# A linear recurrence, a routed expert layer and a second network in one kernel: choice of experts taken into the recurrence

## The chip, the cores and the metric

One core of a Trainium2 chip runs the whole program. The metric is the device time of one execution in microseconds. Engines are written PE (TensorE), DVE (VectorE), ACT (ScalarE), POOL (GpSimd) and SP (SyncE, which here only issues DMAs).

## The reference

Three stages follow each other, with 4 batches x 768 steps = 3072 tokens of 8 heads x 48 = 384 features.

```python
def _attn_ref(q, k, v, alpha):            # q, k, v, alpha: (4, 8, 768, 48)
    for t in range(S):
        state = alpha[:, :, t, :, None] * state + einsum('bhd,bhe->bhde', k[:, :, t], v[:, :, t])
        y[:, :, t] = einsum('bhd,bhde->bhe', q[:, :, t], state)

def _moe_ref(x, expert_emb, tau, w1, w2):  # x (3072, 384), 8 experts, w1 (8, 384, 1024), w2 (8, 1024, 384)
    logits = normalised(x) @ normalised(expert_emb).T / tau
    expert_idx = argmax(logits, axis=1)
    gate_w = softmax(logits)[expert_idx]
    out[mask_e] = gate_w * (relu(x[mask_e] @ w1[e]) @ w2[e])

def _moe2_ref(x, w_in, w_out):             # w_in (384, 2048), w_out (2048, 384)
    h = x @ w_in
    return max(0.01 * h, h) @ w_out
```

## The kernel before

**Recurrence.** Tokens are cut into 24 tiles of 128 steps (6 chunks of time x 4 batches, tile n = 4 chunk + batch). Each engine runs its own program; semaphores tie them together. For a tile DVE makes the running products of alpha forward and backward (`prepare`, L788 to L796: scan, reciprocal, scan), POOL multiplies them into q and k (L517 `qt`, L522 `kt`), PE makes the scores (L1133) and turns the keys (L1139), DVE masks the scores (L804), PE multiplies with the values (L1168), makes the outer products for the state (L1188) and adds the part from the old state (L1176), DVE adds up the state (L823), POOL scales it (L530), ACT copies, PE turns the result back and projects it on the expert embeddings (L1148), ACT copies rows and logits (L625, L626) and SP stores the rows to HBM. All engines are one or two tiles apart in a fixed order: PE's step is scores of n+1, projection of n-1, values, outer products and from-state of n; DVE's is prepare of n+2, mask of n+1, state of n; POOL's is prepare of n+2, then the scaling of the state of n-1. DVE's scan of tile n+2 waits for the scaled state of n-2 (L787). The first and the last chunks are written out, those between run in a loop.

**Choice of experts.** It stands between the recurrence and the first expert matmul. When all 24 tiles are through, DVE finds for every token the largest logit (L885 to L906), PE counts and ranks the tokens of each expert (L1220, L1221), DVE lays out 31 windows of 128 slots, each window with tokens of one expert (L919 to L985), then it marks for each tile which slot a token takes (L995 to L1000), POOL multiplies gate values into the marks (L549), and PE sums the marks over the tiles, 24 matmuls (L1226), which gives for every slot its token and its gate. POOL gathers the rows of a window from HBM by these indices (L564).

**Windows.** A window's rows are turned (L1240), multiplied with w1 in two halves of 9 matmuls each (`hidden`, L1249), ReLU, turned (L1260), and multiplied with w2 in 24 matmuls (`contract`, L1269). Every operand is split into a rounded part (ACT) and a rest (DVE: L1037 for x, L1053 for h, L349 for the weights, in six pieces per expert), with three matmuls per product. DVE multiplies the result with the gate (L1065), and POOL scatters the rows to HBM (L585). PE's order is: hidden half of the next window, turn of this one's h, other hidden half, turn of the rows of the one after, contraction.

**Second network.** Rows come back from HBM, six groups of 512 tokens, L1319 and L1326.

## Time and profile before

| | us |
|---|---|
| median of three runs | 882.3 (879.5 to 883.55) |
| profiled execution | 880.55 |
| its span, first to last instruction | 878.7 |
| PE busy | 836.8 |
| PE weight loads | 751.6 |
| DVE busy | 419.7 |
| ACT busy | 334.2 |
| POOL busy | 160.1 |
| from one window's contraction to the next | 9.55 |
| DMA engines, busy share of 30 to 120 us | 0.79 to 0.91 |

Busy time of PE contains the filler matmuls of L1124, and matmul ends are modelled. "Idle before" in a row stands in brackets: how long the engine was idle and who ended it. L numbers are lines of the kernel. The timeline gives start and duration; the chain of waits follows the work that ended last back to its releasers.

### The profile page before, as it was taken

What the parts mean: (1) busy time and instruction counts of PE and PEld (TensorE: products, weight loads), DVE (VectorE), ACT (ScalarE), POOL (GpSimd) and SP (SyncE); (2) the same over time, 40 slices, a digit from 0 to 9 for tenths busy, and PEclk for the clock granted to TensorE, in tenths of its full rate; (3) what the DMA queues carried; (4) which work ended last, traced back from release to release, by engine and by line L of the source; (5) the groups of instructions that cost most, each with busy time, mean ns of one, the idle gap of its engine ahead of it and who ended that gap; (6) DMA issues with size and microseconds to landing.
All of it is one profiled execution on the core that took longest, in us unless ns stands there. A gap on an engine that the chain in (4) does not pass through costs nothing.

```text
span 878.7 us, 17061 instructions
## 1 busy us (share of the span) xinstructions
PE 836.8 (95%) x5435; PEld 751.6 (86%) x5436; DVE 419.7 (48%) x643; ACT 334.2 (38%) x624; POOL 160.1 (18%) x216
## 2 busy tenths in 40 slices
PE   7999974899999999999997999999999999999998
PEld 6888854699999999999985999998998999999997
DVE  7788849444455253455244343343343343343332
ACT  2455443334435344444333333333333333333323
POOL 5566623222222222322210000000000000000000
PEclk7999995899999999999998999999999999999999
DMA  9898860552453351553305000200200300100100
GB/s 220 200 215 207 198 207 0 180 180 65 159 179 123 103 179 32 192 179 105 106 2 107 1 1 25 49 1 6 66 0 0 72 0 0 37 1 1 37 1 36
DMA packets 45265, 76.24 MB, mean 87 GB/s; under 512 B 16231, under 2 KB 35731, under 8 KB 45232
## 3 DMA queue, kind: packets, MB, share of 16 engines
q1 hardware_dynamic: 41264, 64.98, 26.6%
q0 software_dynamic: 3968, 10.82, 3.5%
q8 instruction: 20, 0.33, 0.2%
q14 instruction: 13, 0.11, 0.0%
HBM read 61.63 MB, written 15.53 MB: 88 GB/s over the span
## 4 chain that ended last, share of the span: by engine, by line
PE 84%; issue 4%; DVE 4%; POOL 3%; DMA 2%; SPq 1%; ACT 0%; POOLq 0%; DVEq 0%
PE bank L1326 23%; PE bank L1319 23%; PE bank L1269 15%; PE bank L1249 14%; PE bank L1260 3%; POOL kt L522 1%; PE bank L1240 1%; DVE decay L788 1%; PE bank L1148 1%; PE bank L1133 1%; PE bank L1168 1%; DMA xg<-x_rows,isrc 1%; DVE inv L796 1%; POOL state L530 1%; DMA taus<-tau 1%
## 5 line engine op out<-in xcount | busy, mean ns | idle before, releaser
L1319 PE MATMUL bank<-yT,wts 128*128 128x512 f32 x864 | 217.0, 396 | 6.1 <-DVE yT L1082 6.1
L1326 PE MATMUL bank<-wts,gs 128*128 128x384 f32 x1152 | 217.3, 337 | 0.0
L1326 PEld LDWEIGHTS bank<-wts,gs 128*128 128x128 f32 x1152 | 204.4, 188 | 8.9 <-issue 0.4
L1319 PEld LDWEIGHTS bank<-yT,wts 128*128 128x128 f32 x864 | 161.9, 189 | 36.6 <-DVE yT L1082 6.9
L1100 DVE TENSOR_TENSOR g<-bank,small 128x512 f32<-128x512 f32 x96 | 66.4, 691 | 180.6 <-ACT small L743 180.6
L1249 PE MATMUL bank<-wts,gxT 128*128 (+1 forms) x558 | 143.2, 401 | 1.2 <-DVE gxT L1037 1.2
L1269 PE MATMUL bank<-wts,hT 128*128 x744 | 137.3, 339 | 1.6 <-DVE hT L1053 1.6
L1269 PEld LDWEIGHTS bank<-wts,hT 128*128 128x128 f32 x744 | 128.5, 188 | 1.9 <-issue 1.8
L743 ACT ACTIVATE small<-bank 128x512 f32<-128x512 f32 x96 | 57.3, 597 | 191.0 <-PE bank L1319 190.9
L1249 PEld LDWEIGHTS bank<-wts,gxT 128*128 128x128 f32 x558 | 103.0, 190 | 20.9 <-DVE gxT L1037 1.5
L1102 DVE TENSOR_TENSOR gs<-g,gs 128x512 fp32r<-128x512 f32 x96 | 66.4, 692 | 67.0 <-ACT gs L746 67.0
L746 ACT ACTIVATE gs<-g 128x512 fp32r<-128x512 f32 x96 | 60.7, 632 | 72.7 <-DVE g L1100 72.7
L690 ACT ACTIVATE hT<-bank 128x512 fp32r<-128x512 f32 x62 | 33.6, 595 | 126.7 <-PE bank L1260 126.7
L349 DVE TENSOR_TENSOR wts<-raw,wts 128x1024 f32 (+1 forms) x60 | 69.9, 1220 | 18.7 <-ACT wts L343 18.7
L585 POOL DMA_INDIRECT y_rows<-ys,idst x31 | 32.2, 1040 | 198.6 <-DVE ys L1065 198.6
L1053 DVE TENSOR_TENSOR hT<-bank,hT 128x512 fp32r<-128x512 f32 x62 | 39.9, 686 | 53.9 <-ACT hT L690 53.9
L343 ACT ACTIVATE wts<-raw 128x1024 f32 (+1 forms) x60 | 58.9, 1056 | 2.5 <-PE bank L1269 2.5
L1065 DVE TENSOR_SCALAR ys<-bank,slot_gate 128x384 f32<-128x384 f32 x31 | 19.0, 614 | 47.4 <-PE bank L1269 47.4
L1037 DVE TENSOR_TENSOR gxT<-bank,gxT 128x384 fp32r<-128x384 f32 x31 | 17.3, 557 | 47.6 <-ACT gxT L669 47.6
L673 ACT ACTIVATE hs<-bank 128x512 f32<-128x512 f32 x62 | 37.2, 601 | 7.1 <-PE bank L1249 7.1
L564 POOL DMA_INDIRECT xg<-x_rows,isrc x31 | 33.5, 1081 | 28.1 <-POOL isrc L558 27.0
L517 POOL TENSOR_TENSOR qt<-qkas,decay 112x512 f32<-112x512 f32 x24 | 30.6, 1275 | 40.4 <-DVE decay L788 40.4
(155 smaller groups left out, 676.9 us busy)
## 6 DMA issues: line engine op xcount, KB each, us to landing
raw<-w SPq DMA_DIRECT2D x14, 1536.0 KB, 7.1
qkas<-qka SPq DMA_DIRECT2D x40, 289.5 KB, 4.8
vs<-v SPq DMA_DIRECT2D x24, 192.0 KB, 4.7
x_rows<-xs SPq DMA_DIRECT2D x24, 192.0 KB, 4.5
yl<-y_rows SPq DMA_DIRECT2D x24, 192.0 KB, 4.4
out<-os SPq DMA_DIRECT2D x5, 768.0 KB, 4.3
raw<-w_in SPq DMA_DIRECT2D x2, 1536.0 KB, 6.8
raw<-w_out SPq DMA_DIRECT2D x2, 1536.0 KB, 7.3
```

The costliest lines, as they stand in the source:

```text
L343: act.activation(set_of(par, 0, cols), raw[:, cols], ACT.Copy).then_inc(w_hi, 1)
L349: dve.tensor_tensor(set_of(par, 1, cols), raw[:, cols], set_of(par, 0, cols).bitcast(F32), ALU.subtract).then_inc(w_lo, 1)
L673: act.activation(hs[:, u, half * HALF:(half + 1) * HALF], hps[u][half][:, :], ACT.Relu).then_inc(relu_done, 1)
L743: act.activation(small[:, f % 2], gps[f % 2][:, :], ACT.Copy, scale=0.01).then_inc(small_done, 1)
L746: act.activation(gs[:, f % 4, 0], g[:, f % 2], ACT.Copy).then_inc(g_hi, 1)
L1053: dve.tensor_tensor(hT[:, 1, h], htps[half][:, :], hT[:, 0, h].bitcast(F32), ALU.subtract).then_inc(ht_lo, 1)
L1100: dve.tensor_tensor(g[:, f % 2], gps[f % 2][:, :], small[:, f % 2], ALU.max).then_inc(g_done, 1)
L1102: dve.tensor_tensor(gs[:, f % 4, 1], g[:, f % 2], gs[:, f % 4, 0].bitcast(F32), ALU.subtract).then_inc(g_lo, 1)
L1249: m = pe.matmul(hps[u][half][:, :], gxT[:, u, x_part, k * P:(k + 1) * P], set_of(par, w_part, slice(n, n + HALF)), start=(k == 0 and (x_pa ...
L1269: m = pe.matmul(yeps, hT[:, h_part, k * P:(k + 1) * P], set_of(par, w_part, slice(n, n + D)), start=(k == 0 and (h_part, w_part) == (0, 0) ...
L1319: m = pe.matmul(gps[f % 2][:, :], wts[:, 0, w_part, n:n + P], yT[:, u, y_part, k], start=(k == 0 and (w_part, y_part) == (0, 0)), stop=(k ...
L1326: m = pe.matmul(ops[tt], gs[:, f % 4, g_part, tt * P:(tt + 1) * P], wts[:, 1, w_part, f * D:(f + 1) * D], start=(f == 0 and (g_part, w_par ...
```

## The change

The choice of experts is spread over the recurrence, and the gate moves to the end.

- The loops over tiles are written out. POOL scales the state of tile n-1 before it prepares tile n+2.
- tau goes into the embeddings, so that logits come out ready. DVE runs `route` for groups of four tiles (the last four tiles are two groups of two) at tiles 5, 9, 13, 17, 21 and after the end: best expert of each token, and a scan that counts on from the groups before. PE sums the ranks (`rank_group`), and DVE's `rank` turns them into a place in the expert's own list (3072 places per expert).
- POOL's `mark` makes two one-hot arrays per tile, 128 x 192 for the list's column and 128 x 128 for the row times token number. PE sums them over four tiles (`list_chunk`), DVE adds this to what it has (`add_listed`). The result holds each expert's tokens in columns of 128.
- After 16 tiles DVE picks the expert with most tokens (`choose_first`). Its weights are loaded first, experts follow in cyclic order, and two windows of it are sure. Their rows are gathered when the lists of 16 tiles are there, near the end of the recurrence. Turn, hidden layer and contraction of windows 0 and 1 are written out by hand between the last tiles, routes, ranks and lists.
- The layout of windows (`lay_out`, `encode`) runs on one partition. The gate is computed after the second window (`weigh`) and applied at the very end by ACT as it copies the output (scale of `os_`); DVE's L1065 becomes a plain copy.
- Tokens are stored in the order of tiles, and `o_grp` undoes it. Many tiles of the recurrence lie in the memory of the second weight set. PSUM banks 6 and 7 change roles.

```diff
-        MADE = 9
-        SLOT_TILES = 6
+        MADE = 3
+        TABLES = 13
-        START_BUSY, GATHER_BUSY, Y_BUSY = 12, 10, 26
+        START_BUSY, Y_BUSY = 12, 26
+        ROUTE_AT = {BATCHES * (g + 1) + 1: g for g in range(CH - 1)}
+        RANK_AT = {n + 1: g for n, g in ROUTE_AT.items()}
+        MARK_AT = {t + 7: (t,) for t in range(12)} | {19: (12, 13), 20: (14, 15)}
+        LIST_AT = {BATCHES * c + 11: c for c in range(3)} | {21: 3}
...
@@ sync
+            for n in range(TILES - BATCHES):
+                refill_qka(n + 2)
+                sp.wait_ge(tile_done, n + 1)
+                load_v(n + BATCHES)
+                if n > 0:
+                    store_x(n - 1)
+                if n == TILES - BATCHES - 2:
+                    sp.wait_ge(first_known, 1)
+                    expert0 = sp.value_load(est[0:1, 0:1], min_val=0, max_val=E - 1)
+                    load_first(0, expert0)
+                    load_first(1, expert0)
+            for part in range(2, PIECES):
+                load_first(part, expert0)
...
@@ gpsimd
+            def mark(t):
+                pool.wait_ge(pos_ready, group_of(t) + 1)
+                wait_from(pool, list_summed, (t - HOTS) // BATCHES + 1)
+                pool.tensor_scalar(list_hot[:, t % HOTS], list_at[:, :], pos[:, 1, t:t + 1], None,
+                                   ALU.is_equal).then_inc(list_marked, 1)
+                pool.tensor_scalar(row_hot[:, t % HOTS], row_at[:, :], pos[:, 2, t:t + 1], token[:, t:t + 1],
+                                   ALU.is_equal, ALU.mult).then_inc(list_marked, 1)
+            for n in range(TILES):
+                if 0 < n <= TILES - BATCHES:
+                    scale_state(n - 1)
+                if n + 2 < TILES:
+                    prepare(n + 2)
+                for t in MARK_AT.get(n, ()):
+                    mark(t)
+            wait_stored(SURE * BATCHES)
+            pool.wait_ge(members_ready, 1)
+            for w in range(2):
+                fetch(w, EARLY)
+            for t in range(SURE * BATCHES, TILES):
+                mark(t)
...
@@ vector
+            def route(g):
+                dve.wait_ge(lg_copied, tiles[-1] + 1)
+                dve.tensor_reduce(lg, lgq[:, r0:r0 + G], AX.X, ALU.add).then_inc(lg_summed, 1)
+                dve.tensor_copy(heads[G][:, :, 0], source)
+                dve.wait_ge(lg_summed, g + 1)
+                link(dve.tensor_reduce(top, lg, AX.X, ALU.max))
+                link(dve.tensor_tensor(some, lg, over(top), ALU.is_equal))
+                link(dve.tensor_tensor(some, some, prio[:, :].unsqueeze(1).to_broadcast([P, G, E]), ALU.mult))
+                link(dve.tensor_reduce(most, some, AX.X, ALU.max))
+                link(dve.tensor_tensor(heads[G][:, :, 1:].rearrange("p e c -> p c e"), some, over(most), ALU.is_equal))
+                dve.tensor_tensor_scan(flat(sums[G][:, :, :]), flat(marks[G][:, :, :]), flat(heads[G][:, :, :]), 0.0,
+                                       ALU.mult, ALU.add).then_inc(hot_ready, 1)
+            def take_members():
+                dve.wait_ge(list_added, SURE)
+                expert0 = dve.value_load(est[0:1, 0:1], min_val=0, max_val=E - 1)
+                dve.tensor_scalar(members[:, 0:2], so_far[:, ds(expert0 * (CAP // P), 2)], float(N), None,
+                                  ALU.add).then_inc(members_ready, 1)
...
+            for n in range(TILES):
+                if n + 2 < TILES:
+                    prepare(n + 2)
+                if n + 1 < TILES:
+                    mask(n + 1)
+                if n in ROUTE_AT:
+                    route(ROUTE_AT[n])
+                if n < TILES - BATCHES:
+                    advance(n)
+                if n in LIST_AT:
+                    add_listed(LIST_AT[n])
+                if n == TILES - 2:
+                    take_members()
+                    split_lo(dve, 0, 0, [0])
+                if n in RANK_AT:
+                    rank(RANK_AT[n])
+                if n == SURE * BATCHES + 2:
+                    choose_first()
+            split_lo(dve, 0, 0, [1])
+            route(CH - 1)
             gx_rest(0, 0)
-            split_lo(dve, 0, 0, range(4, PIECES))
+            split_lo(dve, 0, 0, [2])
+            add_listed(CH - 2)
+            rank(CH - 1)
             gx_rest(1, 1)
+            route(CH)
+            split_lo(dve, 0, 0, [3])
+            rank(CH)
+            lay_out()
+            split_lo(dve, 0, 0, [4])
+            for half in range(2):
+                ht_rest(0, half)
+            split_lo(dve, 0, 0, [5])
+            add_listed(CH - 1)
+            encode()
+            take_y(0, 0)
+            split_lo(dve, 1, 1, W1_PIECES)
+            for half in range(2):
+                ht_rest(1, half)
+            gx_rest(2, 0)
+            split_lo(dve, 1, 1, W2_PIECES)
+            take_y(1, 1)
+            gx_rest(3, 1)
+            weigh()
...
@@ tensor
+            for n in range(TILES):
+                if n + 1 < TILES:
+                    scores(n + 1)
+                else:
+                    turn_gx(0, 0)
+                if n > 0:
+                    turn_and_project(n - 1)
+                values(n)
...
+            pe.wait_ge(gx_lo, 1)
             hidden(0, 0, 0, 0)
+            turn_and_project(TILES - 1)
+            list_chunk(CH - 2)
+            rank_group(CH - 1).then_inc(rank_ready, 1)
             turn_gx(1, 1)
             hidden(0, 0, 0, 1)
+            rank_group(CH).then_inc(rank_ready, 1)
+            hidden(1, 1, 0, 0)
+            turn_h(0, 0)
+            hidden(1, 1, 0, 1)
+            list_chunk(CH - 1)
+            pe.wait_ge(w_lo, PIECES)
+            contract(0, 0, 0)
+            turn_h(1, 1)
+            pe.wait_ge(ys_ready, 1)
+            contract(1, 1, 0)
+            turn_gx(2, 0)
```

`rank` is five dependent DVE steps on 128 x 32 and smaller, `choose_first` five on 128 x 8, `lay_out` a register read and 13 dependent steps on one partition (four of them on 192 to 217 elements), `encode` some 12 on 31 elements, `weigh` 8, an Exp on ACT, and 3.

## Rows read from the trace of the kernel before

**Rows 1.** Timeline, one tile: start us, duration, engine, line, operation, [idle before <-releaser].

```profile
99.50 1.28 POOL L522 TENSOR_TENSOR kt<-qkas,inv 112x512 f32<-112x512 f32 x1 [0.20 <-DVE inv L796]
...
100.74 0.51 POOL L530 TENSOR_TENSOR state<-state_sum,decay 112x192 f32<-112x192 f32 x1
...
101.36 1.22 DVE L788 TENSOR_TENSOR_SCAN decay<-qkas,bank 112x512 f32<-112x512 f32 x1 [0.30 <-POOL state L530]
...
102.92 1.22 DVE L796 TENSOR_TENSOR_SCAN inv<-qkas,bank 112x512 f32<-112x512 f32 x1
...
104.06 1.26 DVE L804 TENSOR_TENSOR probs<-bank,causal 128x512 f32<-128x512 f32 x2
...
105.23 0.34 DVE L823 TENSOR_TENSOR state_sum<-state,bank 112x192 f32<-112x192 f32 x1
```

**Rows 2.** Chain of waits, a tile on PE: start us, duration, what.

```profile
86.82 1.16 PE bank L1133 x16
...
90.43 0.36 PE bank L1188 x16
...
91.44 1.16 PE bank L1133 x16
```

**Rows 3.** Timeline: scans of tiles 4 and 22, last from-state product.

```profile
25.94 1.21 DVE L788 TENSOR_TENSOR_SCAN decay<-qkas,bank 112x512 f32<-112x512 f32 x1
...
110.81 1.22 DVE L788 TENSOR_TENSOR_SCAN decay<-qkas,bank 112x512 f32<-112x512 f32 x1 [0.53 <-POOL state L530]
...
126.71 0.66 PE L1176 MATMUL bank<-qt,state 48*48 48x128 f32 x16
```

**Rows 4.** Timeline: small dependent steps on DVE.

```profile
17.30 0.14 DVE L831 TENSOR_SCALAR embn<-embn 8x1 f32<-8x1 f32 x1
17.48 0.15 DVE L832 RECIPROCAL embn<-embn 8x1 f32<-8x1 f32 x1
```

**Rows 5.** Timeline: one-input select, then products and compares of 192 elements.

```profile
2.18 0.28 POOL L498 TENSOR_SCALAR_AFFINE_SELECT not_before<-not_before 128x128 f32<-128x128 f32 x1
...
140.57 0.36 DVE L995 TENSOR_TENSOR decay<-count,posf 128x192 f32<-128x192 f32 x1
...
141.00 1.28 POOL L549 TENSOR_TENSOR wts<-decay,gate_hi 128x192 fp32r<-128x192 f32 x1 [21.48 <-DVE decay L995]
...
142.25 0.62 POOL L549 TENSOR_TENSOR wts<-decay,gate_lo 128x192 fp32r<-128x192 f32 x1
142.42 0.66 DVE L995 TENSOR_TENSOR decay<-count,posf 128x192 f32<-128x192 f32 x1
```

**Rows 6.** Timeline, first gather and its turn; chain of waits, second gather.

```profile
152.89 1.24 POOL L564 DMA_INDIRECT xg<-x_rows,isrc  x1 [1.08 <-issue]
...
156.34 0.52 PE L1240 MATMUL bank<-ident,xg 128*128 128x128 f32 x3 [1.37 <-DMA xg<-x_rows,isrc]
...
156.23 7.41 DMA xg<-x_rows,isrc
```

**Rows 7.** Timeline, first windows; the last two lines are from the chain of waits.

```profile
151.79 4.63 DVE L349 TENSOR_TENSOR wts<-raw,wts 128x1024 fp32r<-128x1024 f32 x4
...
158.08 3.91 PE L1249 MATMUL bank<-wts,gxT 128*128 128x512 f32 x9 [1.23 <-DVE gxT L1037]
...
164.79 0.56 DVE L1037 TENSOR_TENSOR gxT<-bank,gxT 128x384 fp32r<-128x384 f32 x1 [4.49 <-ACT gxT L669]
...
169.54 1.29 DVE L1053 TENSOR_TENSOR hT<-bank,hT 128x512 fp32r<-128x512 f32 x2 [4.20 <-ACT hT L690]
...
185.45 2.08 PE bank L1249 x9
190.82 4.19 PE bank L1269 x24
```

**Rows 8.** Busy table: stretch, length, busy us (count) per engine, PE clock, DMA share, GB/s.

```profile
128.00:132.00 4.00, 1.12 (x8) 0.97 (x8) 1.59 (x8) 3.25 (x11) 0.00 (x0) 0.86 0.31 114
...
468.00:472.00 4.00, 0.45 (x1) 0.45 (x2) 2.46 (x4) 1.22 (x2) 0.00 (x0) 0.60 1.23 211
```

## What the change does to the time, predicted

> **What bounds the kernel now.** I read three stages out of the views. The busy table by stretch and the timeline show a recurrence up to 128 us, a stretch without MoE matmuls up to 158 us, 31 windows up to 460 us, and the second network. In the last two TensorE (PE) is the bound: one contraction of 24 matmuls ends at 195.0 [rows 7], and the next ones follow at 9.55 us each (the profile table). The change adds nothing to the PE work of a window and leaves the second network's loops alone, so I carry everything to one mark, the end of the contraction of window 2, at 190.82 + 4.19 = 195.0 us. After it both kernels run the same work.
>
> In the recurrence two limits lie close together. The chain of waits shows stretches that are all PE: from the scores of one tile at 86.82 to those of the next at 91.44 are 4.62 us, and the outer products L1188 end 3.96 us into a tile [rows 2]. The timeline shows the other, a ring over two engines: GpSimd (POOL) kt 1.28, state 0.51, then VectorE (DVE) decay scan, reciprocal and inverse scan, 2.78 us from 101.36 to the end at 104.14, then kt again [rows 1]. That ring is 4.6 us of work with small gaps. The scans start at 25.94 (tile 4) and 110.81 (tile 22), so a tile takes 84.87 / 18 = 4.72 us [rows 3]. A reader should see that DVE itself, 2.78 + 1.26 for the mask + 0.34 for the state = 4.4 us less its overlaps, 4.2 [rows 1], has only half a microsecond left per tile.
>
> The last from-state product begins at 126.71 and is over at 127.4 [rows 3]. From there to the mark are 67.6 us, in which PE has some 33 us of work (three contractions at 4.19, four windows of hidden layer at 2 x 2.08 = 4.16, and for turns the 1.2 per window that 9.55 leaves) [rows 7]. The remaining 34 us are the choice of experts, which is one chain of small DVE steps, the marking of 24 tiles, the gather, and a low clock. That is what the change goes for.
>
> **Recurrence, part by part.** The change puts work on an engine with little room. Linked small DVE steps follow each other at 0.18 us (17.30 to 17.48) [rows 4]; I take 0.2. A route of four tiles is 8 steps, one of them a reduction over 128 elements: 1.7 us. A rank is 5 steps: 1.0 us. Adding a list, 192 elements from PSUM, is 0.35 us by the 0.36 of the 192-element compare [rows 5]. So 3.05 us of DVE per four tiles. PE gets two small matmuls and four of 192 columns per four tiles, about 0.8 us. POOL gets two marks per tile: between 0.28 each (the one-input select of 128 elements) and 1.28 + 0.85 (the two-input product of 192, and two thirds of it) [rows 5]. I take 0.7, near the select, since a mark too has one tensor input. POOL is at 0.51 for the state and about 1.28 each for qt and kt, 3.1 us of a tile [rows 1], so 0.7 fits.
>
> One thing gets better: POOL now scales the state before it prepares the tile after next, so DVE's scan no longer waits for kt through the state. The ring is open, and the base falls to the 4.62 of PE.
>
> The routes lie between mask and state update. I follow one group, counting from PE's start of a tile. Normally DVE starts its step at -0.2, masks at 2.5 to 3.8 and updates the state at 4.4. In the route's tile the update ends at 5.9; the next mask ends 2.78 + 1.26 later, at 5.3 of the following tile instead of 4.6. With the rank behind it the tile after is late by 0.7 again, and the list's tile by 0.2. The group costs PE 4 x 4.62 + 1.9 = 20.4 us, against 4 x 4.72 = 18.9. The first of four groups finds slack and costs 1.0, two cost 1.5, the last 2.2 with the 1.0 us choice of the first expert. So R = 6.2 us by the scan of tile 22, T = 110.8 + 6.2 = 117.0. The bounds of R: 2 us if only DVE's sum counts less slack, 18 below.
>
> Removed loops (the code of all 24 tiles now stands in a row) I cost at nothing: the chain has no gap that recurs with the loop's four tiles beyond 0.2 us. The additional tables POOL makes at the start lie in its wait for the first scan and loads. Loads of the first expert's weights now wait for the choice in SyncE's queue, with x stores and v loads behind them; they have some 17 us until they are needed.
>
> **From T to the mark.** All in us after T. DVE does two tiles of 2.78 + 1.26, a route and a list: 10.2. The mask of tile 23: 11.5. It reads the number of the first expert into a register and takes its rows. The nearest row for a register read is the 1.08 of "issue" before the first gather [rows 6]; I take 1.0 and 0.2, to 12.7. The gather took 3.45 us from its issue (152.89) to the turn (156.34) with the queues empty, and 7.4 us the second time [rows 6]. I take the first, since the first expert's 3 MB should be nearly in: G = 16.2. PE has been idle from about 12, because turn_gx(0) stands in its queue before the projection of tile 22 and the values of tile 23.
>
> Behind it come that projection, values and from-state (19.3), the copies and the third piece of weights, which ScalarE and DVE can only split after them (22.3), the rest of the first hidden half (23.0), projection 23, a list and its addition (24.9), a rank (26.4). Then DVE, in order: gxT rest 0.56, route 1.7, split 1.16, rank 1.0, the window layout with one register read and 13 linked steps, nine at 0.2 and four wide ones at 0.36, 4.3 together; split 1.16, two hT rests 1.29, split 1.16 [rows 4, 5, 7]. That is 12.3 after 26.4: contraction 0 may start at 38.7, while PE's own work is done at 34.7. It ends at 42.9. Contraction 1 waits for y taken 0.6, three splits 3.5 and half of the hT rests 0.7: from 47.7 to 51.9. Turn, round and rest of window 2 end at 53.5; hidden 2 and 3 with turns (8.3 + 1.5) end at 63.3; contraction 2 ends at 67.5. The gate's arithmetic (some 12 steps and an Exp) hides behind hidden 3, to within 0.5. If that cover is gone it costs 4.
>
> The mark is at 117.0 + 67.5 = 184.5 against 195.0: 10.5 us earlier. The 6.2 us of R are in it.
>
> **Clock.** This order leaves three PE waits of about 4 us (before G, before contraction 0, before contraction 1). In the trace the granted clock is 0.86 over 128 to 132, when PE had gone quiet, and 0.60 over 468 to 472, in which PE was busy for 0.45 us [rows 8]. These are mixes of its levels, 2.4 and 1.2 GHz. Work after such a fall is dear: 9 matmuls took 3.91 us at 158.08 instead of 2.08 [rows 7], 1.8 us lost. Three waits cost 0 to 6 us; I take 3.5, since each wait is short and it may not fall in all. The old start's own loss is in the 195.0.
>
> The Trainium skill ("TensorE: Matmul & The Clock Gate", HAM oscillation) says that waits between bursts of matmuls make the clock fall again and again and that each burst pays for it. This speaks against the change; by it all three would pay, and the gain would be 10.5 - 6 = 4.5 us. The two falls in this trace agree in kind, and no row shows a gap of 4 us.
>
> **Sum.** 10.5 - 3.5 = 7.0 us less. The profiled execution took 880.55 us (span 878.7), so 873.55; the median of the runs, 882.3, lies 1.75 higher: 875.3 us.
>
> **Rivals.** A measurement here tells about 0.5% (4.4 us) from no change.
> (a) The clock holds and the linked steps are cheaper than 0.2 us, so that R is 2: the mark is at 112.8 + 67.5 = 180.3 and the gain 14.7 us: 867.6. For it: none of the three waits is as long as the stop behind the fall at 468 to 472. Against: DVE has some 30 dependent steps more in the recurrence's groups.
> (b) The first gather goes like the second of the old kernel, 7.4 us, because the 3 MB of weights started only two to four tiles earlier: +4.0 on the same path, 879.3, no difference to be told. For it: the DMA engines are busy for 0.8 to 0.9 of the time up to 120 us (the profile table). Against: 20 us pass from the first of these loads to the gather.
> (c) Slower: POOL and DVE get in each other's way in the recurrence. The place is the marks beside the routes. The trace has it: the same product of 192 took POOL 1.28 beside DVE and 0.62 alone, and DVE's compare 0.36 alone and 0.66 beside POOL [rows 5]. If DVE's 3.05 us of additions become 5.6 and marks 2.1, POOL needs 5.4 us per tile; R becomes 18 and the mark comes at 110.8 + 18 + 67.5 + 3.5 = 199.8: 4.8 us later, 887.1. It decides from 7.0 us on, that is when the additions cost 4.8 per group instead of 3.05. Against it: kt took no more than 1.28 beside scan and mask, each of which has an input in PSUM [rows 1].
> The Trainium skill ("GPSIMD Engine Reference", Specifications) states this contention for DVE operations with two SBUF inputs or in a two-port mode; the trace agrees with 1.28 against 0.62. By it only the short route steps collide, which makes (c) unlikely.
> (d) It doesn't do what it says, if the first window's rows came only after the recurrence. The order of the queues excludes it, except as (b).
>
> **Chances.** Forecast 0.50, (a) 0.15, (b) 0.18, (c) 0.17. About a tenth of the forecast's share falls into no difference. Faster 0.60, same 0.22, slower 0.18. The range from 866 to 889 takes in (a), (b), (c) and the 0 to 6 us of the clock.
>
> **What would show it.** Tiles 5 to 20 at 5.0 us instead of 4.72, with PE waiting for masks behind route and rank; POOL marks of 0.3 to 0.4 us each; the first turn of gathered rows about 16 us after the scan of tile 22, PE idle before it; contraction 0 released by the last split on DVE; contraction 2 ending near 188; the span behind it unchanged, 683.7 us. I am wrong if the recurrence's tiles lengthen by over 0.7 us or not at all, if the PE waits add up to much more than 12 us, or if windows from the third on take other than 9.55 us.

## The result and the profile after

The changed kernel takes **920.7 us** (median of 4 runs, 917.29 to 923.03) against 882.2 us for the kernel before (4 runs, 879.5 to 883.55): a ratio of 1.044, 95% interval 1.0409 to 1.0472. I had forecast 875.3 us. The profiled execution has a span of 919.8 us against 878.7 us, so there are 41.1 us to place.

The page of the changed kernel gives the first hint. Below are its line of busy times, two lines of the chain that ended last (shares of the span by engine, then by line), and three of its costliest groups.

```profile
span 919.8 us, 16474 instructions
...
PE 861.2 (94%) x5449; PEld 767.8 (83%) x5450; DVE 427.3 (46%) x706; ACT 334.3 (36%) x623; POOL 185.4 (20%) x233
...
PE 68%; DMA 11%; DVE 6%; issue 6%; POOL 4%; ACT 2%; DVEq 1%; ACTq 1%; POOLq 1%; SPq 1%
PE bank L1433 22%; PE bank L1426 21%; PE bank L1349 9%; PE bank L1329 7%; DMA xg<-x_rows,members 5%; DMA y_rows<-ys,members 5%; PE bank L1211 2%; PE bank L1230 2%; POOL kt L564 1%; DVE wts L374 1%; PE bank L1340 1%; PE bank L1196 1%; POOL qt L558 1%; PE bank L1297 1%; ACT wts L368 1%
...
L1349 PE MATMUL bank<-wts,hT 128*128 (+1 forms) x744 | 151.1, 363 | 9.9 <-DVE hT L1032 6.5
...
L634 POOL DMA_INDIRECT y_rows<-ys,members x31 | 32.2, 1038 | 119.3 <-DVE ys L1037 115.5
...
L590 POOL DMA_INDIRECT xg<-x_rows,members x31 | 34.2, 1102 | 32.9 <-POOL members L618 25.2
```

Two small transfers, the gather `xg<-x_rows` and the scatter `y_rows<-ys`, hold 5% of the span each. A chain of work does not pass through a transfer that is hidden. In the kernel before PE held 84% of the chain and all DMA 2%.

To place the loss I divide the span at two contractions, as the prediction did at one. "Contraction n" is the group of 24 matmuls of window n.

| stretch | before | after | difference |
|---|---|---|---|
| start to the end of contraction 2 | 195.0 | 192.73 + 4.50 = 197.2 | +2.2 |
| from there to the end of contraction 30 | 264.5 | 301.5 | **+37.0** |
| from there to the end | 419.2 | 421.1 | +1.9 |

Nine tenths of the loss lie in the windows, which I had called the same work in both kernels. The timeline shows one of seven such places (start, duration, engine, line, operation, and in brackets the idle time before it and what released it).

```profile
202.16 0.18 POOL L618 COPY members<-everyone 128x1 int32 x1 [2.40 <-DMA y_rows<-ys,members]
203.20 1.05 POOL L590 DMA_INDIRECT xg<-x_rows,members  x1 [0.86 <-POOL members L618]
...
218.33 9.79 SPq L410 DMA_DIRECT2D raw<-w  x2
219.40 1.02 POOL L634 DMA_INDIRECT y_rows<-ys,members  x1 [5.66 <-DVE ys L1037]
...
226.00 0.63 POOL L618 COPY members<-everyone 128x1 int32 x1 [5.57 <-DMA y_rows<-ys,members]
227.49 1.15 POOL L590 DMA_INDIRECT xg<-x_rows,members  x1 [0.86 <-POOL members L618]
...
234.75 0.87 PE L1297 MATMUL bank<-ident,xg 128*128 128x128 f32 x3 [3.50 <-DMA xg<-x_rows,members]
235.27 5.82 PE L1349 MATMUL bank<-wts,hT 128*128 x24
```

Read it from top to bottom. POOL copies the row numbers of a window into one of four columns, `members`, and gathers with them. The copy for window w + 3 overwrites the column of window w - 1, so it waits until the scatter of w - 1 has landed, and that is the scatter that POOL has just issued (`wait_scattered(pool, w + 1, 1 - j % 2)` in POOL's loop over windows). The kernel before has a wait in this loop too, but it stands behind the gather and asks only for the scatter of window w - 2. At 202.16 that costs 2.4 us and nobody notices. At 219.40 the scatter is issued just after a load of expert weights (218.33, two pieces of 1.5 MB). POOL resumes only at 226.00, 6.6 us after the issue. The gather, issued at 227.49, is turned by PE at 234.75, 7.3 us later. PE had nothing to do for 3.5 us, and the contraction behind it takes 5.82 us instead of 4.5: the granted clock is 0.50 from 236 to 238 us, and was 1.00 up to 234. In the waits of the stretch 200 to 500 us (total, times, longest) the same two transfers appear:

```profile
POOL members L618 <- DMA y_rows<-ys,members: 101.7, 24, 6.3
...
PE bank L1297 <- DMA xg<-x_rows,members: 22.4, 7, 3.5
```

The distances between contractions add up to the loss: 9.64 us in a window without a stop, against 9.55 before, which gives 28 x 0.09 = 2.5 us; and seven stops of 3.4 to 5.4 us each, 34.6 together, of which 22.4 are PE's waits of the row above. The other 12.2 are matmuls at a lower clock: behind contraction 2 PE is busy for 277.65 us at a mean clock of 0.97, and for 265.44 us at 1.00 in e1 below, with the same matmuls. The sum is 37.1, the difference in the table 37.0.

### The profile page after: what moved, and what is told of

It reads as the page before. It is cut to its first block, busy times and chain, and to the rows that moved or that the text cites. A ratio compares the mean times of both kernels' runs of the same rounds, so it can differ in the third digit from the quotient of the medians.

```text
span 919.8 us, 16474 instructions
## 1 busy us (share of the span) xinstructions
PE 861.2 (94%) x5449; PEld 767.8 (83%) x5450; DVE 427.3 (46%) x706; ACT 334.3 (36%) x623; POOL 185.4 (20%) x233
## 4 chain that ended last, share of the span: by engine, by line
PE 68%; DMA 11%; DVE 6%; issue 6%; POOL 4%; ACT 2%; DVEq 1%; ACTq 1%; POOLq 1%; SPq 1%
PE bank L1433 22%; PE bank L1426 21%; PE bank L1349 9%; PE bank L1329 7%; DMA xg<-x_rows,members 5%; DMA y_rows<-ys,members 5%; PE bank L1211 2%; PE bank L1230 2%; POOL kt L564 1%; DVE wts L374 1%; PE bank L1340 1%; PE bank L1196 1%; POOL qt L558 1%; PE bank L1297 1%; ACT wts L368 1%
## 5 line engine op out<-in xcount | busy, mean ns | idle before, releaser
L1433 PEld LDWEIGHTS bank<-wts,gs 128*128 128x128 f32 x1152 | 202.0, 188 | 11.1 <-issue 1.8
L1349 PE MATMUL bank<-wts,hT 128*128 (+1 forms) x744 | 151.1, 363 | 9.9 <-DVE hT L1032 6.5
L1349 PEld LDWEIGHTS bank<-wts,hT 128*128 128x128 f32 x744 | 141.8, 204 | 12.2 <-issue 8.4
L634 POOL DMA_INDIRECT y_rows<-ys,members x31 | 32.2, 1038 | 119.3 <-DVE ys L1037 115.5
L1037 DVE COPY ys<-bank 128x384 f32<-128x384 f32 x31 | 17.2, 554 | 62.0 <-PE bank L1349 62.0
L590 POOL DMA_INDIRECT xg<-x_rows,members x31 | 34.2, 1102 | 32.9 <-POOL members L618 25.2
L688 ACT ACTIVATE gxT<-bank 128x384 fp32r<-128x384 f32 x31 | 15.2, 491 | 68.2 <-PE bank L1297 68.2
L692 ACT ACTIVATE hs<-bank 128x512 f32<-128x512 f32 x62 | 37.2, 601 | 5.9 <-PE bank L1329 5.9
```

The lines of the kernel that those rows point to most:

```text
L692: act.activation(hs[:, u, half * HALF:(half + 1) * HALF], hidden_at(w, u, half), ACT.Relu).then_inc(relu_done, 1)
L1349: m = pe.matmul(yeps, hT[:, h_part, k * P:(k + 1) * P], set_of(par, w_part, slice(n, n + D)), start=(k == 0 and (h_part, w_part) == (0, 0) ...
L1433: m = pe.matmul(ops[tt], gs[:, f % 4, g_part, tt * P:(tt + 1) * P], wts[:, 1, w_part, f * D:(f + 1) * D], start=(f == 0 and (g_part, w_par ...
```

## The experiments

All ratios are to the kernel before on the same chip (its median there 880.0 to 880.2 us).

| run | us | ratio, 95% interval |
|---|---|---|
| e1 changed kernel, eight columns | 882.8 | 1.0024 (1.0002 to 1.0046) |
| e2 before, with the wait | 925.2 | 1.0484 (1.0447 to 1.0521) |
| e3 before, tile loops written out | 884.9 | 1.0048 (1.0031 to 1.0065) |
| e4 e3, state scaled first | 878.8 | 0.9985 (0.9970 to 1.0000) |
| e5 e1, PE waits of the last tiles filled | 879.7 | 0.9992 (0.9982 to 1.0002) |
| e7 before, state scaled first | 877.4 | 0.9974 (0.9962 to 0.9987) |
| e8 e4, but POOL keeps its loop | **873.05** | 0.9923 (0.9907 to 0.9940) |
| e9 e5, waits before contractions 0 and 1 filled too | 876.6 | 0.9965 (0.9950 to 0.9979) |
| e10 e9, rows at the old addresses | **873.3** | 0.9924 (0.9911 to 0.9936) |
| e11 before, rows 32 bytes further | 880.5 | 1.0006 (0.9997 to 1.0015) |

**Is it the wait?** Two runs: the changed kernel without it, and the kernel before with it. In e1 `members` has eight columns, so that nothing has to be waited for.

```diff
-    IDS = 4
+    IDS = 8
...
-                    if not first:
-                        wait_scattered(pool, w + 1, 1 - j % 2)
...
-            with pool.Fori(0, (WINDOWS - 3) // IDS - 1) as i:
+            with pool.Fori(0, (WINDOWS - 7) // IDS) as i:
```

> The changed kernel with eight index columns in place of four, and without POOL's wait for the scatter of window w-1 before it takes the column of window w+3. Theory W: this wait is what the windows lost by. In the trace of the changed kernel contraction 2 ends at 197.2 and contraction 30 at 498.7, 301.5 us, against 264.5 before. With the wait gone this stretch is 265 to 267 us again, PE waits for gathered rows nowhere behind window 3, and the time is 920.7 - 36 = 884 to 886 us. Rival X: the windows are slow because taking a column by a register, copying it and gathering is a longer chain on POOL (2.1 us) or because scatters without a gate load the DMA queues differently; then the seven stalls stay and the time is over 905.

Measured: 882.8 us, 38 us less than the changed kernel and 1.2 below the range expected. From the end of contraction 2 to the end of contraction 30 it takes 266.7 us, every window 9.64. The reverse, e2, adds one line to the kernel before and leaves the rest of the change out:

```diff
                     pool.wait_ge(gx_turned, w + 2)
+                    wait_scattered(pool, w + 1, 1 - u, pool_turns)
                     gather(w + 3, 1 - u, w * 2 + 4)
```

> The kernel before with one wait added: POOL waits for the scatter of window w-1 to have landed before it copies the indices and issues the gather of window w+3. Nothing else differs. Theory W: the same stalls appear, the contraction of some windows waits 3 to 5 us for its gathered rows while a weight load is in flight, and the time rises by 25 to 40 us to 907 to 922. Rival X: it rises by less than 5 us, since the old chain of copy and gather is short.

Measured: 925.2 us, 45 us more than before and 3 above the range expected. From the end of contraction 2 to the end of contraction 30 it takes 301.75 us, 37.2 more than before, where the changed kernel takes 37.0 more; another 7.7 us are lost ahead of that, 6.4 of them because here the first stop comes already at contraction 2. The timeline of e2 has the same picture as the changed kernel:

```profile
180.17 1.02 POOL L586 DMA_INDIRECT y_rows<-ys,idst  x1 [12.90 <-DVE ys L1066]
...
186.06 1.17 POOL L558 COPY isrc<-slot_src 128x1 int32 x1 [4.86 <-DMA y_rows<-ys,idst]
188.14 1.12 POOL L564 DMA_INDIRECT xg<-x_rows,isrc  x1 [0.92 <-POOL isrc L558]
...
195.37 0.90 PE L1241 MATMUL bank<-ident,xg 128*128 128x128 f32 x3 [3.61 <-DMA xg<-x_rows,isrc]
```

Scatter, its landing, copy, gather, and a PE wait of 3.61 us. One line makes the loss in a kernel that has nothing else of the change, and taking it out removes it. This is the cause of the 38 us, shown from both sides.

**What did the rest of the change bring?** Without the wait it brings nothing: the ratio is 1.0024, and its interval lies just above 1. Yet it reaches the end of contraction 2 at 188.23 + 4.50 = 192.7, 2.3 us earlier than before; 2.2 us are lost again in the windows (266.7 against 264.5) and 2.2 behind them (421.4 against 419.2). The next runs take its recurrence apart. e3 only writes out the loops over tiles in the kernel before; e4 also swaps the two steps of POOL.

```diff
         def each_tile(eng, step, apart=1):
-            for b in range(BATCHES):
-                step(0, b)
-            with eng.Fori(1, CH - apart) as c:
-                for b in range(BATCHES):
-                    step(c, b)
-            for c in range(CH - apart, CH):
+            for c in range(CH):
                 for b in range(BATCHES):
                     step(c, b)
```

> The kernel before with the loops over the recurrence's tiles written out on all engines, order unchanged. My prediction cost this at nothing: then 882. The trace of the changed kernel has tiles of 4.48 us from scores to scores on PE where the chain before had 4.62, though its tiles do the same matmuls. If that is the loops' register work, this kernel gains up to 0.14 x 16 = 2.2 us where PE is the bound, so 880, and nothing where the ring over POOL and DVE binds.

Measured: 884.9 us, slower by 0.5%, where I had expected 880 to 882. The tiles did get shorter, from 4.72 to 4.66 us, and contraction 0 starts 1.8 us earlier (169.65). But contraction 2 starts at 192.73, 2.2 us late, and takes 6.68 us.

```diff
-                if within(after[0]):
-                    prepare(*after)
                 if within(before[0]) and not is_last(before[0]):
                     scale_state(*before)
+                if within(after[0]):
+                    prepare(*after)
```

> As the previous one, and POOL scales the state of tile n-1 before it prepares tile n+2. The prediction's claim: DVE's scan no longer waits for kt by way of the state, and the tile falls from 4.72 us to PE's own time. With PE's time 4.48 this is 16 x 0.24 = 3.8 us less than before, 878; with 4.62 it is 1.6 less, 880.5. Rival: POOL's scaling now waits for DVE's and PE's step of the same tile in front of qt and kt, and the kernel gets slower than the previous one by 1 us or more.

Measured: 878.8 us. Tiles are down to 4.48 us in their steady run (4.41 on average between the scans of tiles 4 and 22), and contraction 0 starts at 163.96, 7.5 us earlier than before. Of these only 3.0 are left at the start of contraction 2 and 1.4 at its end, since it takes 6.0 us. That the time still met the 878 expected is luck: the start gained more than I had reckoned, and the delay took it back. Here are POOL's first scatters of e3 and e4:

```profile
182.42 1.45 POOL L580 DMA_INDIRECT y_rows<-ys,idst  x1 [18.41 <-issue]
```

```profile
176.73 1.44 POOL L580 DMA_INDIRECT y_rows<-ys,idst  x1 [17.89 <-issue]
```

Their data, `ys`, began to be copied by DVE at 175.53 and 169.85. Each scatter is issued 6.9 us later. In the kernel before the two times are 177.36 and 178.91, 1.5 us apart. The releaser is "issue", so POOL waited for nothing that the profile shows. Two more runs tell whether the swap or the written-out program does it: e7 has the swap alone, e8 has the swap and writes the loops out on all engines but POOL.

> The kernel before with one edit: POOL scales the state of tile n-1 before it prepares tile n+2. The loops stay. If the ring over POOL and DVE was the bound beside PE, tiles go from 4.72 to PE's 4.55 to 4.62 us, and contraction 0 starts 2 to 4 us earlier than at 171.5. If the five lost microseconds between the first y rows and their scatter, which both written-out kernels have, come from the longer programs, they don't appear here, and the time is 2 to 4 us less than before: 877 against 880. If they come from the shifted moment at which the weight load starts, they appear here too, and the time is no less than before.

Measured: 877.4 us, as expected. Tiles take 4.50 us; the scatter at 175.34 follows its `ys` (173.78) by 1.6 us, and contraction 2 starts on time.

```diff
+            if apart == 0:
+                for c in range(CH):
+                    for b in range(BATCHES):
+                        step(c, b)
+                return
...
-            each_tile(pe, step)
+            each_tile(pe, step, 0)
```

The last two lines stand for the same edit on SyncE, ScalarE and DVE; POOL's call is left.

> The written-out kernel with POOL scaling first, but POOL's own loop kept, all other engines written out. In the earlier one POOL began the first scatter 6.9 us after its rows were ready, with nothing awaited in the profile (17.9 us of issue), while 1.5 MB of weights came in; in the kernel before it took 1.5 us. If POOL's longer program is the cause (its instructions are fetched late), the scatter follows at 1.5 us here, contraction 2 isn't late, and the time is 4 us below the 878.8 of the earlier one: 874 to 875, faster than both kernels. Rival: the gap depends on the moment of the weight load, and stays: 879.

Measured: **873.05 us**, a little under the 874 to 875 expected and the fastest of all, and none of it comes from moving the choice of experts: e8 leaves that where it was. The scatter is issued 1.6 us after its `ys` (169.78), and the bracket names DVE again:

```profile
171.35 1.02 POOL L590 DMA_INDIRECT y_rows<-ys,idst  x1 [12.49 <-DVE ys L1070]
```

So POOL's own long program delays its first scatter, and the other engines' do not. That the missing time is the fetch of instructions is argued, not shown: the instruction queue carries 20 packets before and 28 in e3, but 28 in e8 too. The changed kernel has POOL's tiles written out as well, and yet its first scatter comes 1.5 us after `ys` (168.49 to 170.01). There a gather of POOL stands shortly ahead of it (167.19); whether that is why, no run shows.

**What does the clock cost?** The table of busy time by stretch of the changed kernel (length, busy us of PE, weight load, DVE, ACT, POOL, then the granted clock, DMA share, GB/s), and rows of DVE, POOL and PE at the place:

```profile
108.00:112.00 4.00, 3.78 (x44) 3.29 (x44) 3.55 (x13) 1.62 (x5) 2.34 (x5) 1.00 0.41 135
112.00:116.00 4.00, 2.55 (x49) 2.01 (x48) 4.00 (x6) 1.72 (x6) 3.79 (x4) 0.92 0.77 224
116.00:120.00 4.00, 4.00 (x30) 3.40 (x32) 3.90 (x7) 0.18 (x1) 4.00 (x6) 0.50 1.00 348
...
132.00:136.00 4.00, 4.00 (x29) 3.35 (x32) 1.64 (x4) 0.00 (x0) 2.24 (x2) 0.50 0.14 33
136.00:140.00 4.00, 3.60 (x27) 2.77 (x23) 1.24 (x6) 2.94 (x7) 2.95 (x5) 0.50 0.36 120
140.00:144.00 4.00, 4.00 (x38) 3.13 (x38) 2.63 (x10) 2.12 (x6) 3.81 (x5) 0.67 0.14 49
144.00:148.00 4.00, 2.66 (x18) 2.08 (x16) 1.22 (x1) 0.80 (x2) 0.00 (x0) 1.00 0.00 0
```

```profile
108.18 0.18 DVE L921 TENSOR_TENSOR hits<-bank,heads 128x32 f32<-128x32 f32 x1
...
110.53 1.22 DVE L856 TENSOR_TENSOR_SCAN decay<-qkas,bank 112x512 f32<-112x512 f32 x1
```

```profile
113.30 1.27 POOL L564 TENSOR_TENSOR kt<-qkas,inv 112x512 f32<-112x512 f32 x1 [0.21 <-DVE inv L864]
```

```profile
114.63 1.46 PE L1196 MATMUL bank<-qt,kt 48*128 48x128 f32 x16 [1.45 <-POOL kt L564]
```

DVE works out the ranks and the first expert from 108.18 to 110.53, and only then the scans of tile 21; POOL's `kt` follows them, and PE waits 1.45 us for it. The clock falls to its lower level, 1.2 GHz, at 115.35. It stays there for 27 us although PE is busy nearly all the time, with small matmuls at half speed, and is back at 2.4 GHz at 142.66, 0.2 us ahead of the first 512-column matmul. So it wasn't the large matmuls that brought it back. e1 shows the same: behind a wait of 1.46 us at the same place its clock fell at 114.64, and it was back at 118.05 among small matmuls. The table by single microseconds, the changed kernel and then e1:

```profile
142.00:143.00 1.00, 1.00 (x19) 0.80 (x18) 0.77 (x3) 0.00 (x0) 1.00 (x2) 0.67 0.12 40
```

```profile
117.00:118.00 1.00, 1.00 (x12) 0.99 (x10) 1.00 (x3) 0.00 (x0) 1.00 (x2) 0.50 1.00 370
118.00:119.00 1.00, 1.00 (x24) 0.58 (x20) 0.97 (x2) 0.00 (x0) 1.00 (x2) 0.97 0.97 363
```

Why one fall lasted 3.4 us and the other 27 stays open. e1 had a second fall, from 131.7 to 138.5, which began in a wait of 2.59 us for the gathered rows. e5 gives PE needless 128-column matmuls ahead of the last three tiles and of the first turn; e9 also fills the waits before contractions 0 and 1 with 13 matmuls of 512 columns each.

```diff
             for n in range(TILES):
+                if n >= TILES - BATCHES:
+                    keep_busy((8, 2, 2, 8)[n - TILES + BATCHES], bank[6][:, 0:P], ones[:, :], ones[:, :])
```

> The changed kernel with eight index columns (as in the first experiment) and filler matmuls on PE in the last four tiles: 8 before the scores of tile 21, 2 and 2 before those of 22 and 23, 8 before the first turn of gathered rows. They fill waits of PE and change no result. Theory C: the tail and the start of the windows are long because PE's clock fell to 1.2 GHz when PE waited for tile 21 (0.50 from 116 to 140 in the changed kernel) and small matmuls don't bring it back. With the waits filled the clock stays at 2.4 GHz to the first turn, contraction 0 starts 3 to 5 us earlier against the scan of tile 22 than in the first experiment (43.3 us behind it there), and the time falls by 2 to 5 us to 878 to 881. Rival D: the stretch is bound by DVE's order of small steps whatever the clock is; then contraction 0 stays at 43 us behind that scan and the time at 883.

Measured: 879.7 us, 3.1 less than e1. The clock is 1.00 in each stretch of 4 us from 112 to 140, and contraction 0 starts at 155.16 instead of 157.10. The time is in the range expected, but against the scan of tile 22 contraction 0 gained only 2.2 us (41.05 behind it instead of 43.3), not 3 to 5. In the changed kernel it was 47.6 behind, so the long fall there cost 6.5 and the two short ones of e1 2.2.

```diff
             list_chunk(CH - 1)
+            pe.wait_ge(lg_copied, TILES)
+            keep_busy(13, bank[7][:, :], wts[:, 0, 0, 0:P], wts[:, 0, 0, 0:HALF])
             pe.wait_ge(w_lo, PIECES)
             contract(0, 0, 0)
             turn_h(1, 1)
             pe.wait_ge(ys_ready, 1)
+            keep_busy(13, bank[7][:, :], wts[:, 0, 0, 0:P], wts[:, 0, 0, 0:HALF])
             contract(1, 1, 0)
```

> As the filled tail, and 13 filler matmuls of 512 columns each before contraction 0 and before contraction 1. In the first experiment both contractions took 6.0 to 6.9 us at a fallen clock where 4.5 is usual. Theory C: both take 4.5 us now, 3.5 to 4 us less than in the filled tail alone, if the fillers end before the waits do. Rival D: the waits that follow on DVE (y rows, splits, rests) swallow it, and the gain is under 1.5 us.

Measured: 876.6 us, 3.1 less than e5, a little under the 3.5 to 4 expected. The first two contractions of the changed kernel, and those of e9:

```profile
162.43 6.03 PE L1349 MATMUL bank<-wts,hT 128*128 128x384 f32 x24 [3.48 <-DVE wts L374]
...
173.20 2.10 PE L1349 MATMUL bank<-wts,hT 128*128 128x384 f32 x6 [3.87 <-DVE hT L1032]
```

```profile
154.16 4.50 PE L1349 MATMUL bank<-wts,hT 128*128 128x384 f32 x24 [0.45 <-DVE wts L374]
163.32 4.50 PE L1349 MATMUL bank<-wts,hT 128*128 128x384 f32 x24 [0.76 <-DVE hT L1030]
```

The engine and line that release them are the same, and the waits are now filled; the clock is 1.00 from 28 to 200 us. Together the fillers of e5 and e9 bring 6.2 of e1's 882.8 us.

**Why 9.64 us and not 9.55?** The address of the gathered rows was left as a cause. In the kernel before `gxT` begins at byte 143488 of a partition and in the changed one at 143392, 32 off a multiple of 64. e10 puts 96 bytes ahead of `xg` in e9 (and 32 behind `members`), e11 puts 32 bytes ahead of `xg` in the kernel before.

```diff
         est = keep("est", [P, 1], I32)
+        pad = keep("pad", [P, 24])
```

> The kernel of e9 with 96 bytes of padding per partition ahead of xg and 32 behind members, so that xg, gxT, hs and hT begin at the SBUF addresses that they have in the kernel before (143488 for gxT, a multiple of 64); in the changed kernel they begin 32 bytes off such a multiple (143392). The second network's yT and gs keep their remainder. What is open is why every window of the changed kernel takes 9.64 us instead of 9.55, with the same matmuls. Theory P (placement): matmuls that read gxT and hT as weights are slower by 3 ns each when these begin off a multiple of 64 bytes: windows go back to 9.55 us, 28 of them give 2.5 us, 874.1 us against the 876.6 of e9; contraction matmuls at 339 ns instead of 342, hidden ones at 398 instead of 400. Theory Q: it comes from the new index copy and gather (columns of a list, larger tables): nothing changes, windows 9.64 us, 876.6 us.

> The kernel before with 32 bytes of padding ahead of xg, so that xg, gxT, hs and hT begin 32 bytes off a multiple of 64 as in the changed kernel; nothing else moves. Theory P: windows take 9.64 us instead of 9.55, contraction matmuls 342 ns instead of 339, and the kernel 2.5 us more than before: about 882.7 us, ratio 1.003. Theory Q: windows 9.55 us, ratio 1.000.

Measured: e10 takes **873.3 us**, 3.3 less than e9; e11 takes 880.5 us, no more than the kernel before, where theory P had 882.7. PE's groups from 240 to 440 us (count, busy us, mean ns), e9 and then e10:

```profile
L1329 PE MATMUL bank<-wts,gxT 128*128 x372 | 95.3, 400 | 0.0
L1349 PE MATMUL bank<-wts,hT 128*128 x501 | 93.5, 342 | 0.0
```

```profile
L1331 PE MATMUL bank<-wts,gxT 128*128 x377 | 95.9, 398 | 0.0
L1351 PE MATMUL bank<-wts,hT 128*128 x504 | 93.1, 339 | 0.0
```

The windows of e10 are back at 9.55 us, exactly, so the address does make the 0.09 us: 2.4 us from the end of contraction 2 to the end of contraction 30. But the rule that I had put up, a multiple of 64, fell with e11: there windows take 9.57 us, not 9.64, with the same remainder of 32. Placement matters; which property of it does stays open. The second network is 1.7 us shorter in e10 as well (its tensors moved by 128 bytes), which no expectation had named.

## Why the prediction was wrong

**The step that failed** is in the first paragraph: "After it both kernels run the same work." It was made from PE's loops alone. The change rewrites POOL's loop over windows too. Its one wait for a scatter moved from behind the gather to ahead of it, and from the scatter of window w - 2 to that of w - 1. I named every queue that a step of the recurrence was moved past and did not do the same for the windows. The kernel before held half of what was needed to price it: a contended gather of 7.41 us [rows 6] and a window of 9.55 us. It shows no landing of a scatter; with the gather's 7.41 taken for both, an estimate, the chain has 14.8 us to go, more than a window. Measured it is 6.6 + 7.3 us where weights are loaded, and it cost 37.0 us. I did write that the forecast is wrong "if windows from the third on take other than 9.55 us"; that sign came: 9.64 us, and seven windows with a stop. None of the four rivals was this one, and 920.7 lies outside 866 to 889.

**The sum up to the mark** has its own errors, which partly cancel. The mark came at 197.2 instead of 188.0.

- *Recurrence.* The scan of tile 22 starts at 114.84, tile 4's at 25.98, so a tile takes 4.94 us (forecast 5.0) and R is 4.0 instead of 6.2. What a group adds was sized well, though its parts were not: PE's scores of tiles 8, 12, 16 and 20 start 19.9 us apart, which is 4 x 4.48 + 2.0, against a forecast of 4 x 4.62 + 1.9. The linked steps on DVE follow each other at 0.21 us, as assumed, but a route covers 2.2 us (101.70 to 103.88) instead of 1.7. The base is what was off: e4 and e7 measure 4.48 and 4.50 us per tile. With the ring still closed, writing out the loops alone gives 4.66 (e3), so most of it comes from scaling the state first, which opens the ring, as the prediction said. It had missed that PE's 4.62 was not yet PE's own time.
- *POOL's marks.* Two take 0.76 + 0.79 = 1.55 us per tile, not 0.7. The nearest row was the product of 192 elements [rows 5], not the select. That row was also misread: the 0.62 us were not "alone", for POOL's product from 142.25 to 142.87 ran beside DVE's compare that starts at 142.42. Only DVE's 0.36 against 0.66 us is a case alone against a case beside.

```profile
93.52 0.76 POOL L578 TENSOR_SCALAR list_hot<-list_at,pos 128x192 fp32r<-128x192 f32 x1
94.26 0.79 POOL L580 TENSOR_SCALAR row_hot<-row_at,pos,token 128x128 fp32r<-128x128 f32 x1
```

  In the changed kernel they fit into POOL's slack: where `kt` is late (113.30, above) it waits for DVE's inverse scan, not behind marks. In e9, with the clock held, the chain of the tail does pass through two marks, at 113.60 and 115.12.
- *Rival (c), contention.* It had forecast R = 18; R was 4.0, and as a forecast (c) falls. But what it describes is there, with POOL's products and not with its marks. In e9 a step of the route on 128 x 32 elements, which else takes 0.19 us, takes 2.56, and ends as POOL's two products end:

```profile
121.85 2.56 DVE L903 TENSOR_TENSOR cand<-lgs,tops 128x32 f32<-128x32 f32 x1
```

```profile
121.86 1.27 POOL L558 TENSOR_TENSOR qt<-qkas,decay 112x512 f32<-112x512 f32 x1
123.10 1.27 POOL L564 TENSOR_TENSOR kt<-qkas,inv 112x512 f32<-112x512 f32 x1
```

  e1, e5 and e10 have it too (2.56, 2.57 and 2.57 us, each ending within 0.1 us of `kt`); in the changed kernel it is a copy of 128 x 8 elements, 1.62 us from 124.45, beside `kt`. In e9 the chain of waits passes through it.
- *Removed loops.* "I cost at nothing" was off on both sides: 0.06 us per tile gained, and in the kernel before a first scatter 6.9 us behind its data instead of 1.5 (e3).
- *From T to contraction 0.* Forecast 38.7, measured 162.43 - 114.84 = 47.6 us. With the clock held (e9: 154.16 - 113.14) it is 41.0, so 6.6 us are the clock and 2.3 something else. The slow step above has that size (2.4 us more than 0.19) and lies on the chain: in e9 the first gather is issued 14.9 us after T, not 12.7. No run takes it away. The releaser was the last split on DVE, as forecast.
- *From contraction 0 to the mark.* Forecast 28.8, measured 34.8, and 31.7 in e9: here 3.1 us are the clock, and 2.9 are in the order of the steps, not taken apart further.
- *The clock.* I took 3.5 of "0 to 6"; it cost 6.6 + 3.1 = 9.7. Of the three waits that I counted the two before contractions 0 and 1 did cost (3.48 and 3.87 us, 6.0 us per contraction instead of 4.5). The one before the first turn of gathered rows isn't there: the clock was already low, PE was late itself, and the turn came 22.0 us after T instead of 16. The fall that cost most came earlier, at a wait of 1.45 us behind the rank and the choice of the first expert, which my 2.2 us for the last group contained without my asking what PE's clock makes of it; and the clock came back only 27 us later. The Trainium skill ("TensorE: Matmul & The Clock Gate", HAM oscillation) says that in a loop which waits between its bursts of matmuls every burst starts at the low clock again; the trace agrees for the two waits before contractions 0 and 1.

With these the forecast of the mark becomes 110.8 + 4.0 + 41.0 + 31.7 + 9.7 = 197.2. Its gain of 7.0 us was in reach only with the clock held and the old addresses: e10, which has both and no wait, is 6.7 us faster than the kernel before (880.0 to 873.3). e8 gets as much (880.2 to 873.05) from the swapped steps and written-out loops, with the choice of experts left in its place. So no run shows that moving the choice is worth anything by itself.

**What held.** The chain of the recurrence, the ring that the new order opens, the releaser of contraction 0, and the first gather with short queues: issued at 133.45, turned at 136.85, 3.4 us against the 3.45 of [rows 6]. Rival (b), a first gather of 7.4 us, fell; so did (a), since R was 4.0, not 2, and the clock did not hold. The span behind the mark did not stay at 683.7; it is 722.6.

## What to carry to other kernels

When a change rewrites a loop, compare its queue instruction by instruction on every engine, also where the bound engine's work is untouched: one wait that chains a gather behind the landing of a scatter can turn two hidden transfers into the bound. Price such a chain with the longest landing that the trace shows beside other loads, not the usual one. And a change that moves work under an engine's idle time must be costed at the clock that this idle time leaves. Last, take a change of several parts apart before you credit its main idea: here two small parts alone (e8) gave as much as the whole at its best (e10).

## What the runs showed of the hardware

- A scatter of 128 rows is over 3.2 to 3.4 us after its issue when little else moves and 6.6 us beside a load of two pieces of 1.5 MB; a gather behind it takes 7.3 us.
- A PE wait of 1.45 us in the midst of small matmuls was followed, 0.7 us after its end, by a fall of the clock to 1.2 GHz. The low stretch lasted 27 us in the changed kernel and 3.4 us in e1, and in both it ended among small matmuls. Waits of 0.59 and 1.05 us a few microseconds later in e1 were followed by no fall.
- A DVE step with two inputs in SBUF took 2.56 instead of 0.19 us beside two products of POOL, and ended with them (e9).
- POOL with its tiles written out issued its first scatter 6.9 us after the data (e3, e4), with its loop kept 1.6 us (e8). In the changed kernel, written out too, it was 1.5 us.
- The same matmuls take 339 or 342 ns depending on where in SBUF the gathered rows and the tensors behind them begin; moving the gathered rows by 96 bytes was worth about 1% of a window, and a shift by 32 bytes elsewhere 0.2%.
